# The last two blocks of a gated scan with two feed-forward layers: 480 and 480 steps in place of 512 and 448

## The chip, the cores and the metric

The kernel runs on one core of one Trainium2 chip. The metric is the device time of one execution in microseconds (us); less is better. PE is TensorE, DVE is VectorE, ACT is ScalarE, POOL is GpSimd, SP is SyncE.

## The reference, cut to what matters

Two sequences of 6080 steps with 256 channels go through a gated scan, then every step's vector goes through two feed-forward layers of width 2048.

```python
# x, f_logit: (2, 6080, 256), float32
sig = 1.0 / (1.0 + np.exp(-f_logit))
f = lower_bound + (1.0 - lower_bound) * sig
for t in range(6080):
    h = f[:, t] * h + (1.0 - f[:, t]) * x[:, t]
    y[:, t] = h
x = y.reshape(12160, 256)
h = np.maximum(x @ w_in1, 0.0)
x = h * h @ w_out1
h = x @ w_in2
g = np.where(h > 0.0, h, np.exp(np.minimum(h, 0.0)) - 1.0)
out = g @ w_out2
```

## The kernel before, in words

**Blocks.** The steps of both sequences are cut into 12 blocks, numbered 0 to 11 (`TAIL` is 11). A block holds the same stretch of steps of both sequences. Blocks 0 to 10 have 512 steps each, block 11 has the 448 that are left. Within a block the scan is done in four pieces (`pieces_of`): for each sequence the first 256 steps (`HALF`) and the rest.

**Phases.** A block goes through layer 1 in a phase `first(i)` and through layer 2 in a phase `second(i)`. The order of phases is written out by hand and is the same on every engine: `first(0), first(1), second(0), first(2), second(1), first(3), ...`, with the middle in a hardware loop, and at the end `second(8), first(10), second(9), first(11), second(10), second(11)`. The first of these phases that lie behind the loop is `second(8)`.

**Steps.** A phase has 8 steps, one for each pair of 128-wide slices of the hidden layer. In a step PE makes seven products for the current pair ("m1" to "m7", a scheme in which seven products stand for the eight of a 2x2 block product; results in four banks of PSUM, `ring`) and eight products that take the pair of two steps ago down into the sums `acc`. Each of the 15 products is a `triple` of three matmuls (line 626), because each operand is split into a high and a low part. So a step has 45 matmuls, each 128 x 128 against as many columns as the block has steps. The pieces alternate: m1, down, m2, down, and so on, with two products of `acc` side by side at the end of a step. The step of the current pair and the pair of two steps ago may belong to different phases: the first two steps of a phase take down pairs of the phase before.

**The other engines.** ACT and DVE take the seven products out of PSUM, combine and activate them and split the result (`hid_hi`, `hid_lo`); POOL helps. Phases of layer 1 also host, on DVE and ACT, the scan of the next block (`turn_f`, `turn_x`, `tanh`, `gate_x`, `scan`); `first(10)` so hosts the scan of block 11, and `first(11)` hosts none. SP loads the weights of every pair anew, the inputs, and stores the output.

**The end.** Behind `second(11)` stand the downs of the last two pairs (48 matmuls), in an order that suits what arrives last (`END_TILES`, `end_part`). Then DVE transposes `acc` into `o_sb` in five instructions (`end_turn`, line 1719) and SP and ACT store in four pieces (`end_store`, `END_PIECES`); the last of them can start only when the last transpose is done.

**Loop and block 10.** The hardware loop runs with block numbers that are not known when the program is built, and so always with 512 steps. Its last turn hosts part of the load and scan of block 10.

Of the kernel before, what the change touches and what calls it, by code (L numbers as in the profile page):

```python
# [12 lines left out]
SQ = 32  # L13
# [22 lines left out]
def gated_scan_two_ffn(nc, x, f_logit, lower_bound, w_in1, w_out1, w_in2, w_out2, out):  # L36
    B, T, D = x.shape
    F = w_in1.shape[1]
    CH = D // P
    S = BANK  # L40
    N_FULL = T // S
    TAIL = N_FULL
    S_TAIL = T - N_FULL * S
    LAST = 2 * TAIL + 1
    G = P // SQ
    ROWRUN = D // G
    assert CH == 2 and B == 2 and F == PAIRS * 2 * P
    assert HALF < S_TAIL < S and S_TAIL % SQ == 0 and N_FULL >= 4

    def known(i, block):  # L50
        return isinstance(i, int) and i == block

    def steps_of(i):
        return S_TAIL if known(i, TAIL) else S

    @dataclass
    class Phase:
# [6 lines left out]
        def n(self):  # L64
            return steps_of(self.i)
# [11 lines left out]
    def second(n):  # L77
        if known(n, TAIL):
            return Phase(2, n, LAST, PAIRS * LAST)
        return Phase(2, n, 2 * n + 2, PAIRS * 2 * n + 2 * PAIRS)  # L80
# [31 lines left out]
    def early(v):  # L112

        return isinstance(v, int) and v <= 0

    with ExitStack() as ctx:  # L116
        def sb(name, shape, dt=F32):
            return ctx.enter_context(nc.sbuf_tensor(name, shape, dt))
# [4 lines left out]
        def sem(name):  # L123
            return ctx.enter_context(nc.semaphore(name))
# [18 lines left out]
        f_raw = sb("f_raw", [P, CH * HALF])  # L143
        x_raw = sb("x_raw", [P, CH * HALF])
# [55 lines left out]
        f_loaded = sem("f_loaded")  # L200
        x_loaded = sem("x_loaded")
# [132 lines left out]
        def pieces_of(i):  # L334

            return [(b, h * HALF, min(HALF, steps_of(i) - h * HALF)) for b in range(B) for h in range(2)]
# [11 lines left out]


        END_TILES = (1, 0, 2, 3)  # L350
        MID = S_TAIL // SQ // 2
        END_PIECES = ((1, 0, MID), (1, MID, 2 * MID), (0, 0, MID), (0, MID, 2 * MID))

        END_TURNS = (1, 2, 4, 5)

# [7 lines left out]
        out_v = out.rearrange("(b t) d -> b t d", b=B)  # L363

        def end_store(eng, v, parts):

            b, k0, k1 = END_PIECES[v]
            eng.wait_ge(end_turned, END_TURNS[v])
            for a in parts:
                rows = out_v[b, TAIL * S + k0 * SQ:TAIL * S + k1 * SQ, a * ROWRUN:(a + 1) * ROWRUN]  # L370
                i = o_sb[a * SQ:(a + 1) * SQ, b, k0:k1, :, :]
                eng.dma_start(rows.rearrange("(k t) e -> t k e", t=SQ),
                              i.rearrange("t k c e -> t k (c e)")).then_inc(end_stored, DMA_INC)
# [4 lines left out]
        def _(sp):  # L378
# [11 lines left out]
            def load_rows(src, b, t0, n, dst, loaded, parts=range(G)):  # L390
                for a in parts:
                    rows = src[b, bass.ds(t0, n), a * ROWRUN:(a + 1) * ROWRUN]
                    o = dst[a * SQ:(a + 1) * SQ, 0:n * CH]
                    sp.dma_start(o.rearrange("t (k e) -> t k e", e=ROWRUN),
                                 rows.rearrange("(k t) e -> t k e", t=SQ)).then_inc(loaded, DMA_INC)

            def load_f(i, q):
                b, t0, n = pieces_of(i)[q]
                c = 4 * (i - 1) + q
                if not early(c):  # L400
                    sp.wait_ge(f_turned, c)
                load_rows(f_logit, b, i * S + t0, n, f_raw, f_loaded)

            def load_x(i, q):
                b, t0, n = pieces_of(i)[q]
                c = 4 * (i - 1) + q
                if not early(c):
                    sp.wait_ge(x_turned, c)
                load_rows(x, b, i * S + t0, n, x_raw, x_loaded)

            def raw_in_done(layer, p):

# [84 lines left out]
            def store_rows(n, b):  # L497
                S_ = steps_of(n)
                sp.wait_ge(o_n1 if b else o_n0, n + 1)
                for a in reversed(range(G)):  # L500
                    rows = out_v[b, bass.ds(n * S, S_), a * ROWRUN:(a + 1) * ROWRUN]
                    i = o_sb[a * SQ:(a + 1) * SQ, b, 0:S_ // SQ, :, :]
                    sp.dma_start(rows.rearrange("(k t) e -> t k e", t=SQ),
                                 i.rearrange("t k c e -> t k (c e)")).then_inc(out_stored[b], DMA_INC)

            def load_piece(ph, p):

                if p in (1, 4, 6) and not known(ph.i, TAIL):
                    load_f(ph.i + 1, (p + 1) // 2)
                    load_x(ph.i + 1, (p + 1) // 2)  # L510

            def phase(ph, after):
# [8 lines left out]
                for p in range(PAIRS):  # L521
                    g = ph.base + p
                    nxt = ahead(p + 2)
                    if known(ph.order, 0):
                        if p >= 1:
                            if p < PAIRS - 1:
                                load_raw_out(1, p + 1)
                            keep_q(1, p)
                            if 2 <= p < 5:
                                load_f(1, p - 1)  # L530
                                load_x(1, p - 1)
                            keep_sums(1, p - 1)
                            if p + 3 < PAIRS:
                                load_raw_in(1, p + 3)
                            elif p + 3 < PAIRS + 2:
                                load_raw_in(2, p + 3 - PAIRS)
                        if p >= PAIRS - 2:
                            load_s(nxt)
                            load_sums(nxt)
                        if p == 6:  # L540
                            load_f(2, 0)
                            load_x(2, 0)
                        continue
# [29 lines left out]
                    if before is not None and before.layer == 2:  # L573
                        if p == 2:
                            store_rows(before.i, 1)
                        if p == 3:
                            store_rows(before.i, 0)
# [36 lines left out]
            phase(second(TAIL), None)  # L614
            for v in range(len(END_PIECES)):
                end_store(sp, v, (0, 1))
            for b in range(B):
                sp.wait_ge(out_stored[b], DMA_INC * G * TAIL)
            sp.wait_ge(end_stored, DMA_INC * G * len(END_PIECES))

# [279 lines left out]
        def _(act):  # L900
# [424 lines left out]
            def end_hi_of(k):  # L1325
                act.wait_ge(end_elu, END_TILES.index(k) + 1)
                if k == 1:
                    act.wait_ge(down_n1, end.g - 1)
                if k == 2:
                    act.wait_ge(down_n0, end.g - 1)  # L1330
                nc.scalar.activation(hid_hi[:, end.par(), k, 0:end.N], end_x(end, k), ACT.Copy).then_inc(end_hi, 1)
# [8 lines left out]
            end_hi_of(3)  # L1340
            for v in range(len(END_PIECES)):
                end_store(act, v, (2, 3))

        @block.vector
        def _(dve):
# [371 lines left out]
            def end_turn(b, k0, k1, c0, c1):  # L1717

                nc.vector.transpose(o_sb[:, b, k0:k1, c0:c1, :].rearrange("p k c e -> p c k e"),  # L1719
                                    acc[:, b, c0:c1, k0 * SQ:k1 * SQ].rearrange("p c (k e) -> p c k e", e=SQ)).then_inc(  # L1720
                    end_turned, 1)

            dve.wait_ge(end_down, 1)
            dve.wait_ge(out_stored[1], DMA_INC * G * TAIL)
            end_turn(1, 0, MID, 0, CH)
            end_turn(1, MID, 2 * MID, 0, CH)
            dve.wait_ge(end_down, 2)
            dve.wait_ge(out_stored[0], DMA_INC * G * TAIL)
            end_turn(0, 0, 2 * MID, 0, 1)
            dve.wait_ge(end_down, 3)  # L1730
            end_turn(0, 0, MID, 1, CH)
            end_turn(0, MID, 2 * MID, 1, CH)

        @block.gpsimd
        def _(pool):
# [234 lines left out]
```

## Time and profile before

| | us |
|---|---|
| median of three timed runs | 1965.78 (1965.6 to 1966.9) |
| span of the profiled execution | 1963.6 |
| PE busy within the span | 1957.7 |
| DVE busy | 1604.5 |
| ACT busy | 1518.6 |
| POOL busy | 643.5 |

The span runs from the first to the last instruction of the profiled execution; the time of that execution as the timed runs count it is not listed apart. The median of the timed runs is 2.2 us more than the span, and this rest is taken as the same before and after. PE has an instruction in flight in all but 5.9 us of the span, which says that it never starves; it does not say how fast its matmuls follow one another. Matmuls overlap, so the distance between their starts is what counts, and not the duration of one.

### The profile page before, as it was taken

The numbers are of one execution on the slowest core, as the hardware profiler recorded it, in microseconds if no ns is written. First come the engines' busy times: TensorE is split into PE (matmuls) and PEld (weight loads), VectorE is DVE, ScalarE is ACT, GpSimd is POOL, SyncE is SP. The second block draws the span as 40 slices with busy tenths as digits, with TensorE's granted clock in tenths as the row PEclk, the third lists the DMA queues.
The fourth block names the chain that finished last, engine by engine and source line by source line (L and its number), as shares of the span: only waits on it lengthen the run. The fifth ranks groups of instructions, "written<-read, shape, count | busy, mean of one in ns | idle before, by whom it ended". The sixth has DMA issues, their size and how long they took to land.

```text
span 1963.6 us, 27999 instructions
## 1 busy us (share of the span) xinstructions
PE 1957.7 (100%) x8712; PEld 1632.4 (83%) x8712; DVE 1604.5 (82%) x1806; ACT 1518.6 (77%) x1848; POOL 643.5 (33%) x534
## 2 busy tenths in 40 slices
PE   9999999999999999999999999999999999999999
PEld 7888888888888888888888888888888888888888
DVE  7878887888888788888888888888888887866887
ACT  8898877877778777777777877777787777767766
POOL 4666632323223232232322323223232232332311
PEclk9999999999999999999999999999999999999999
DMA  6677453444444445344444444534434443443453
GB/s 196 204 228 227 165 150 106 148 145 127 147 135 125 130 147 146 107 148 136 126 147 142 127 124 144 147 111 150 135 119 148 145 130 113 137 136 118 140 172 112
DMA packets 228679, 281.54 MB, mean 143 GB/s; under 512 B 153857, under 2 KB 164098, under 8 KB 228610
## 3 DMA queue, kind: packets, MB, share of 16 engines
q1 hardware_dynamic: 226688, 280.23, 46.4%
q8 instruction: 35, 0.57, 0.1%
q10 hardware_dynamic: 1922, 0.46, 0.1%
q14 instruction: 34, 0.28, 0.0%
HBM read 248.25 MB, written 32.37 MB: 143 GB/s over the span
## 4 chain that ended last, share of the span: by engine, by line
PE 100%; DVE 0%; DVEq 0%; issue 0%
PE acc L626 53%; PE ring L626 46%; PE ring L663 0%; PE ring L778 0%; PE acc L785 0%; PE acc L663 0%; PE ring L785 0%; DVE o_sb L1719 0%; PE ring L823 0%; DVEq L116 0%; DVE m_sb L1632 0%
## 5 line engine op out<-in xcount | busy, mean ns | idle before, releaser
L626 PE MATMUL acc<-hid_hi,wout 128*128 128x512 f32 (+1 forms) x3072 | 1149.9, 387 | 0.0
L626 PE MATMUL ring<-t_hi,s_w 128*128 128x512 f32 (+1 forms) x2672 | 1027.3, 387 | 0.0
L626 PEld LDWEIGHTS acc<-hid_hi,wout 128*128 128x128 f32 x3072 | 576.8, 188 | 113.4 <-DMA wout<-w_kept 0.2
L626 PE MATMUL acc<-hid_lo,wout 128*128 128x512 f32 (+1 forms) x1536 | 594.7, 387 | 0.0
L626 PEld LDWEIGHTS ring<-t_hi,s_w 128*128 128x128 f32 x2672 | 501.7, 188 | 99.5 <-ACT xb L1182 0.3
L1895 POOL TENSOR_TENSOR xb<-xb,m_sb 128x512 f32<-128x512 f32 (+1 forms) x184 | 236.3, 1284 | 971.4 <-DVE hid_lo L1530 971.4
L626 PE MATMUL ring<-t_lo,s_w 128*128 128x512 f32 (+1 forms) x1336 | 517.2, 387 | 0.0
L1174 ACT ACTIVATE m_sb<-ring 128x512 f32<-128x512 f32 (+1 forms) x184 | 109.2, 593 | 354.1 <-PE ring L626 345.4
L626 PEld LDWEIGHTS acc<-hid_lo,wout 128*128 128x128 f32 x1536 | 288.4, 188 | 56.6
L626 PEld LDWEIGHTS ring<-t_lo,s_w 128*128 128x128 f32 x1336 | 250.9, 188 | 49.6
L1530 DVE TENSOR_TENSOR hid_lo<-xa,hid_hi 128x1024 fp32r<-128x1024 f32 (+1 forms) x191 | 231.3, 1211 | 61.4 <-ACT hid_hi L1153 61.2
L1530 DVE TENSOR_TENSOR hid_lo<-xb,hid_hi 128x1024 fp32r<-128x1024 f32 (+1 forms) x190 | 238.6, 1256 | 5.3 <-ACT hid_hi L1163 5.1
L1163 ACT ACTIVATE hid_hi<-xb 128x1024 fp32r<-128x1024 f32 (+1 forms) x190 | 199.0, 1047 | 38.4 <-DVE xb L1524 38.2
L1572 DVE TENSOR_TENSOR xa<-ring,u_sb 128x1024 f32<-128x1024 f32 (+1 forms) x184 | 221.7, 1205 | 0.0
L1524 DVE SCALAR_TENSOR_TENSOR xa<-ee,xa 128x1024 f32<-128x1024 f32 (+1 forms) x95 | 116.6, 1227 | 110.2 <-ACT ee L1120 110.2
L1153 ACT ACTIVATE hid_hi<-xa 128x1024 fp32r<-128x1024 f32 (+1 forms) x191 | 198.5, 1039 | 0.3
L1555 DVE TENSOR_TENSOR u_sb<-ring,m_sb 128x512 f32<-128x512 f32 (+1 forms) x184 | 123.9, 674 | 50.6 <-PE ring L626 49.4
L1561 DVE TENSOR_TENSOR u_sb<-ring,u_sb 128x512 f32<-128x512 f32 (+1 forms) x184 | 126.2, 686 | 43.9 <-PE ring L626 31.5
L1576 DVE TENSOR_TENSOR xa<-ring,xa 128x512 f32<-128x512 f32 (+1 forms) x184 | 126.3, 686 | 19.1
L1524 DVE SCALAR_TENSOR_TENSOR xb<-ee,xb 128x1024 f32<-128x1024 f32 (+1 forms) x95 | 115.4, 1214 | 23.5 <-ACT ee L1143 23.5
L1580 DVE TENSOR_TENSOR xb<-ring,u_sb 128x512 f32<-128x512 f32 (+1 forms) x184 | 123.5, 671 | 0.0
L1182 ACT ACTIVATE xb<-ring 128x512 f32<-128x512 f32 (+1 forms) x184 | 105.4, 573 | 0.0
(146 smaller groups left out, 1761.0 us busy)
## 6 DMA issues: line engine op xcount, KB each, us to landing
s_w<-s_kept SPq DMA_DIRECT2D x184, 512.0 KB, 3.8
s_w<-s_kept SPq DMA_DIRECT2D x184, 384.0 KB, 4.0
wout<-w_kept SPq DMA_DIRECT2D x88, 512.0 KB, 4.3
out_dram<-o_sb SPq DMA_DIRECT2D x88, 128.0 KB, 3.6
f_raw<-in_f_logit_dram SPq DMA_DIRECT2D x168, 64.0 KB, 3.5
x_raw<-in_x_dram SPq DMA_DIRECT2D x168, 64.0 KB, 2.7
s_kept<-ee SPq DMA_DIRECT2D x16, 512.0 KB, 4.1
s_kept<-s_w SPq DMA_DIRECT2D x8, 512.0 KB, 4.0
```

The lines of the kernel that those rows point to most:

```text
L626: mm = nc.tensor.matmul(out_ap, lhs[a], rhs[b], start=start and t == 0, stop=stop and t == 2)
L1153: nc.scalar.activation(hid_hi[:, pr.par(), 0:2, 0:N], xa[:, pr.par(), :, 0:N], ACT.Copy).then_inc(hi_n1, 1)
L1163: nc.scalar.activation(hid_hi[:, pr.par(), 2:4, 0:N], xb[:, pr.par(), :, 0:N], ACT.Copy).then_inc(hi_n0, 1)
L1174: nc.scalar.activation(m1_sb[:, 0:N], bank("m1", cur), ACT.Copy).then_inc(m1_kept, 1)
L1524: nc.vector.scalar_tensor_tensor(out=x2, in0=ee[:, v, :, 0:pr.N], scalar=1.0, in1=x2, op0=ALU.subtract, op1=ALU.max).then_inc(done, 1)
L1530: nc.vector.tensor_tensor(hid_lo[:, pr.par(), k:k + 2, 0:N], x2, hid_hi[:, pr.par(), k:k + 2, 0:N].bitcast(F32), ALU.subtract).then_inc(do ...
L1555: nc.vector.tensor_tensor(u[:, 0], bank("m6", cur), m1_sb[:, 0:N], ALU.add).then_inc(u2_done, 1)
L1561: nc.vector.tensor_tensor(u[:, 1], bank("m7", cur), u[:, 0], ALU.add).then_inc(u3_done, 1)
L1572: nc.vector.tensor_tensor(t, bank("m5", cur).unsqueeze(1).broadcast_to([P, 2, N]), u, ALU.add).then_inc(u4_done, 1)
L1576: nc.vector.tensor_tensor(t[:, 0], bank("m3", cur), t[:, 0], ALU.add).then_inc(c12_done, 1)
L1580: nc.vector.tensor_tensor(x_n0(cur)[:, 1], bank("m4", cur), u[:, 1], ALU.add).then_inc(c21_done, 1)
L1895: nc.gpsimd.tensor_tensor(t, t, m1_sb[:, 0:N], ALU.add).then_inc(c11_done, 1)
```

## The change

The numbers of steps of the last two blocks are evened out: block 10 has 480 steps instead of 512 and block 11 has 480 instead of 448. Block 11 so starts at step 5600 instead of 5632. Because 480 is 15 times 32, the four end pieces are cut as 8 and 7 groups of 32 steps instead of 7 and 7.

```diff
-    S_TAIL = T - N_FULL * S
+    S_TAIL = (T - (TAIL - 1) * S) // 2
...
     def steps_of(i):
-        return S_TAIL if known(i, TAIL) else S
+        return S_TAIL if known(i, TAIL) or known(i, TAIL - 1) else S
+
+    def start_of(i):
+        return (TAIL - 1) * S + S_TAIL if known(i, TAIL) else i * S
...
-        MID = S_TAIL // SQ // 2
-        END_PIECES = ((1, 0, MID), (1, MID, 2 * MID), (0, 0, MID), (0, MID, 2 * MID))
+        KS = S_TAIL // SQ
+        MID = (KS + 1) // 2
+        END_PIECES = ((1, 0, MID), (1, MID, KS), (0, 0, MID), (0, MID, KS))
...
-            end_turn(1, MID, 2 * MID, 0, CH)
+            end_turn(1, MID, KS, 0, CH)
...
-            end_turn(0, 0, 2 * MID, 0, 1)
+            end_turn(0, 0, KS, 0, 1)
...
-            end_turn(0, MID, 2 * MID, 1, CH)
+            end_turn(0, MID, KS, 1, CH)
```

The other edits put `start_of(i)` where `i * S` stood in the loads and stores. No instruction is added, removed or moved past another on any engine: the five instruction streams are the same before and after but for the lengths. In the phases `first(10)` and `second(10)` 512 becomes 480 (720 matmuls), in `first(11)`, `second(11)` and the end 448 becomes 480 (720 matmuls). The second scan piece of block 11 grows from 192 to 224 steps; that of block 10 is still turned and scanned with 256 steps, since this lies in the loop.

## Rows read from the trace of the kernel before

**Rows 1.** The page: span and the chain that ended last.
```profile
span 1963.6 us, 27999 instructions
PE 100%; DVE 0%; DVEq 0%; issue 0%
```

**Rows 2.** Chain of work in first(10): start, duration, what; step ends three steps apart.
```profile
1565.49 1.36 PE acc L626 x6
...
1596.09 1.36 PE acc L626 x6
```

**Rows 3.** Chain of work in second(11): step ends four steps apart.
```profile
1902.40 1.22 PE acc L626 x6
...
1938.88 1.22 PE acc L626 x6
```

**Rows 4.** Chain of work where phases meet: starts of mixed steps, and what follows.
```profile
1719.85 0.61 PE ring L626 x3
1720.46 0.69 PE acc L626 x3
...
1739.48 0.61 PE ring L626 x3
...
1794.20 0.68 PE ring L626 x3
...
1812.43 1.21 PE acc L626 x6
...
1874.87 0.61 PE ring L626 x3
...
1894.49 0.61 PE ring L626 x3
```

**Rows 5.** Timeline of PE near the start: start, time, instruction.
```profile
7.93 0.64 PE L785 MATMUL acc<-m_sb,xb 128*128 128x128 f32 x4
8.41 1.03 PE L778 MATMUL ring<-m_sb 128*128 128x512 bf16 x4
...
16.28 0.62 PE L663 MATMUL ring<-t_lo,s_w 128*128 128x512 f32 x2
...
19.50 1.07 PE L663 MATMUL acc<-t_hi,s_w 128*128 128x512 f32 x4
```

**Rows 6.** Weight loads from 1905 to 1945 us: busy us, mean ns, idle before.
```profile
L626 PEld LDWEIGHTS acc<-hid_hi,wout 128*128 128x128 f32 x70 | 13.1, 188 | 1.0
```

**Rows 7.** Busy time of each engine in three windows of first(10).
```profile
core 0: us, PE busy (x) PEld busy (x) DVE busy (x) ACT busy (x) POOL busy (x), PEclk, DMA share, GB/s
1576.60:1586.80 10.20, 10.20 (x46) 8.45 (x46) 8.18 (x10) 7.83 (x9) 4.17 (x4) 1.00 0.52 142
1586.80:1597.00 10.20, 10.20 (x46) 8.45 (x46) 10.01 (x12) 8.28 (x11) 3.99 (x4) 1.00 0.50 140
1597.00:1607.20 10.20, 10.20 (x46) 8.45 (x46) 6.53 (x9) 7.83 (x9) 3.71 (x4) 1.00 0.56 145
```

**Rows 8.** DVE in the timeline of first(10), and PE's chain after it.
```profile
1595.92 1.21 DVE L1572 TENSOR_TENSOR xa<-ring,u_sb 128x1024 f32<-128x1024 f32 x1
...
1598.81 0.68 PE ring L626 x3
```

**Rows 9.** DVE groups by form: count, busy us, mean ns, idle before.
```profile
L1572 DVE TENSOR_TENSOR xa<-ring,u_sb 128x1024 f32<-128x1024 f32 x168 | 204.4, 1217 | 0.0
L1561 DVE TENSOR_TENSOR u_sb<-ring,u_sb 128x512 f32<-128x512 f32 x168 | 116.2, 692 | 39.9 <-PE ring L626 28.3 <-issue 0.4
L1572 DVE TENSOR_TENSOR xa<-ring,u_sb 128x896 f32<-128x896 f32 x16 | 17.3, 1084 | 0.0
L1561 DVE TENSOR_TENSOR u_sb<-ring,u_sb 128x448 f32<-128x448 f32 x16 | 10.0, 622 | 4.0 <-PE ring L626 3.2
L1719 DVE STREAM_TRANSPOSE o_sb<-acc 128x448 f32<-128x448 f32 x3 | 1.8, 636 | 1.6 <-PE acc L626 1.6
L1719 DVE STREAM_TRANSPOSE o_sb<-acc 128x224 f32<-128x224 f32 x2 | 0.7, 396 | 0.0
```

**Rows 10.** The end: chain of work, then timeline.
```profile
1948.00 10.43 PE acc L626 x51
...
1951.92 0.62 DVE L1706 TENSOR_TENSOR hid_lo<-xa,hid_hi 128x448 fp32r<-128x448 f32 x1
...
1958.45 1.32 DVE L1719 STREAM_TRANSPOSE o_sb<-acc 128x448 f32<-128x448 f32 x3 [1.25 <-PE acc L626]
1958.65 0.37 PE L626 MATMUL acc<-hid_hi,wout 128*128 128x448 f32 x1
```

More of the change, by code:

```diff
@@ L48, in gated_scan_two_ffn @@
     assert HALF < S_TAIL < S and S_TAIL % SQ == 0 and N_FULL >= 4
+    assert (TAIL - 1) * S + 2 * S_TAIL == T
     def known(i, block):
@@ L369, in end_store @@
             for a in parts:
-                rows = out_v[b, TAIL * S + k0 * SQ:TAIL * S + k1 * SQ, a * ROWRUN:(a + 1) * ROWRUN]
+                rows = out_v[b, start_of(TAIL) + k0 * SQ:start_of(TAIL) + k1 * SQ, a * ROWRUN:(a + 1) * ROWRUN]
                 i = o_sb[a * SQ:(a + 1) * SQ, b, k0:k1, :, :]
@@ L401, in load_f @@
                     sp.wait_ge(f_turned, c)
-                load_rows(f_logit, b, i * S + t0, n, f_raw, f_loaded)
+                load_rows(f_logit, b, start_of(i) + t0, n, f_raw, f_loaded)
             def load_x(i, q):
@@ L408, in load_x @@
                     sp.wait_ge(x_turned, c)
-                load_rows(x, b, i * S + t0, n, x_raw, x_loaded)
+                load_rows(x, b, start_of(i) + t0, n, x_raw, x_loaded)
             def raw_in_done(layer, p):
@@ L500, in store_rows @@
                 for a in reversed(range(G)):
-                    rows = out_v[b, bass.ds(n * S, S_), a * ROWRUN:(a + 1) * ROWRUN]
+                    rows = out_v[b, bass.ds(start_of(n), S_), a * ROWRUN:(a + 1) * ROWRUN]
                     i = o_sb[a * SQ:(a + 1) * SQ, b, 0:S_ // SQ, :, :]
```

## The prediction

> **What bounds the kernel now.** I read the chain of work that ended last first. It says PE for 100% of the span [rows 1]: apart from a short start and the stores at the end, time is the sum of the distances between PE's matmuls, and every other engine waits for PE. So the question is not which engine is late, but what one matmul costs at 512, 448 and 480 columns.
>
> The chain's pieces in order of time give these distances. In the profile's rows a step ends with the only piece of six matmuls in a row, so two such pieces lie whole steps apart. In `first(10)`, with 512 columns, three steps take 1596.09 - 1565.49 = 30.60 us [rows 2], 10.20 us for 45 matmuls, 226.7 ns each. In `second(11)`, with 448 columns, four steps take 1938.88 - 1902.40 = 36.48 us [rows 3], 9.12 us for 45, or 202.7 ns each. The clock that the windows show is 1.00 [rows 7], the 2.4 GHz level; 512 columns at one per cycle would be 213.3 ns and 448 would be 186.7 ns. So a matmul carries 13.3 ns more than its columns at 512, but 16.0 ns more at 448. The overhead is not a constant, and that is what the whole sum hangs on. Were the distance a straight line in the columns, an even split would move nothing.
>
> A third reading is that of steps in which both widths alternate. The two mixed steps of `first(11)` take 1739.48 - 1719.85 = 19.63 us [rows 4]. Each has 21 matmuls of 448 and 24 of 512 columns; at the distances above that is 21 x 0.2027 + 24 x 0.2267 = 9.697 us, 19.39 for two. They are 0.24 us longer, and the rows show where: a triple of 448 takes 0.61 us as ever, one of 512 takes 0.69 instead of 0.68. The two of `second(10)` (21 of 512, 24 of 448) run from 1794.20 to 1812.43 + 1.21, 19.44 us against 19.25; those of `second(11)` from 1874.87 to 1894.49, 19.62 us against 19.39 [rows 4]. All six mixed steps together cost 0.24 + 0.19 + 0.23 = 0.66 us over the pure ones. A 512-column matmul so has a longer distance when it does not stand among its like. The same is seen near the start: 14 matmuls of 512 columns from 16.28 to 19.50 us [rows 5] take 3.22 us, 230.0 ns each, and the timeline marks no idle time ahead of these two rows. 226.7 ns is a favourable rhythm that a long run of 512s has; a run of 448s shows no equal of it.
>
> **The matmuls.** The change touches 1440 of them: 16 steps x 45 = 720 in the two phases of block 10 and as many in those of block 11. Before, they cost 720 x 0.2267 + 720 x 0.2027 = 309.1 us, plus 0.66 us in mixed steps, together 309.8 us. After, they cost 1440 x p, with p the distance at 480 columns, which no row shows. Bounds:
> - From below: 480 columns are 200.0 ns, and the least overhead seen in a long run is 13.3 ns. p = 213.3, 307.2 us. If such a rhythm also survives in the mixed steps, their 0.66 us go too: -2.6 us at most, -1.9 us if they stay.
> - From above: the price per column of the 448s, 202.7 / 448 = 0.4524 ns. p = 217.1 ns, 312.7 us, +3.5 us with the mixed steps as they are.
>
> There are six mixed steps after as before: `first(10)`, `second(9)` and `first(11)` each start with pairs of another width, while `second(10)` and `second(11)` then follow phases of their own width. So I leave the 0.66 us in. 480 lies halfway between the two widths and neither row is nearer, so I take the mean of the two prices per column, (0.4427 + 0.4524) / 2 = 0.4476 ns: p = 214.8 ns. A straight line between the two distances would give 214.7 and a change of nothing. My term is 1440 x 0.2148 = 309.3 against 309.1: **+0.2 us**.
>
> The Trainium skill ("TensorE: Matmul & The Clock Gate", section "Back-to-back issue gap") gives the distance of warm matmuls as columns over 2.4 GHz plus 2.5 ns, a straight line with a fixed overhead. By it the sum of the matmuls would not move at all, as long as the columns are the same in number. The trace does not agree with its fixed part, 13.3 and 16.0 ns here, and it is the difference of these two by which the result can move either way.
>
> **The engines beside PE.** DVE's instructions shrink in block 10 and grow in block 11, all under cover. The one tight place is the third step window of `first(10)`, where DVE hosts scan work of block 11 and is busy 10.01 us of 10.20 [rows 7]. There PE's step shrinks to 45 x 0.2148 = 9.67 us. DVE's seven pair instructions of a step shrink by half of the difference between the two forms: (1217 - 1084) / 2 = 67 ns for each of three wide ones, (692 - 622) / 2 = 35 ns for each of four narrow ones [rows 9], 0.34 us in all, while the second scan piece with 224 instead of 192 steps adds some 0.1 us. So DVE would have 9.8 us of work in a step of 9.67: late by 0.1 us. What waits for it is the next step's second product, which needs line 1572 to have read the banks: it is done at 1595.92 + 1.21 = 1597.13 and the product starts at 1598.81 [rows 8], a margin of 1.7 us. The next window has only 6.53 us of DVE work [rows 7], so the lateness is made good. Cost 0. If that cover were gone, it would be 0.1 us for each such step, at most a few tenths.
>
> In `first(11)`, `second(10)` and `second(11)` the same engines fed steps of 9.12 us without a gap; a step of 9.67 us gives them more time for their fixed costs. Cost 0.
>
> **The end.** The 54 matmuls behind the last product run without a gap (from 1948.00 [rows 10]; three records are missing). Their 24 first cover the chain of the first end tile, whose low part is ready at 1951.92 + 0.62 = 1952.54, while its matmul comes at 1948.00 + 24 x 0.2027 = 1952.86. A margin of 0.3 us. With 480 columns the 24 matmuls take 24 x 0.012 = 0.3 us more, and nine DVE and ACT instructions of that chain, at 35 to 67 ns each, 0.3 to 0.5 us more, but these start a dozen matmuls earlier, which adds another 0.15 us to PE's side. It holds, or is short by at most 0.1 us. Behind the last matmul (1958.65 + 0.37 = 1959.02) DVE is busy until 1958.45 + 1.32 = 1959.77 [rows 10]. The transposes cost (636 - 396) / 224 = 1.07 ns per column [rows 9]; 32 more columns in each of two of these three give 0.07 us. The last store has seven groups as before, the one ahead of it eight instead of seven. Together **+0.1 us**.
>
> The sum: 0.2 + 0.1 = +0.3 us on the span of 1963.6. The median of the runs shown is 1965.78, 2.2 us above the span, and I put the change on it: **1966.1 us**. A measurement of this kernel can tell about 0.2%, 3.9 us, from no change; this is far within.
>
> **The rivals.**
> - *480 finds a rhythm like that of 512* (overhead 13.3 ns). For it: 512 settles in one and stays. One mechanism that gives the same number is a floor from weight loading: each load takes 188 ns [rows 6], and 202.7 ns at 448 could be that floor and 14 ns of handing over, which 480 would clear. Against the floor: four 128-column matmuls with four weight loads take 8.41 - 7.93 = 0.48 us [rows 5], 120 ns each, so loads can come faster than every 202 ns. Sum: -1.9 to -2.6 + 0.1, **1963.3 to 1964.0 us**. Chance 0.25.
> - *480 finds none* (16 ns as for 448 up to 17.1 ns, the same price per column). For it: 448s keep that price through 16 steps, 512s out of rhythm pay nearly the same per column, 230.0 / 512 = 0.449 ns. Against: nothing but the midpoint. Sum: 1440 x (0.2160 to 0.2171) - 309.1 = +1.9 to +3.5, with the end **1967.8 to 1969.4 us**. Chance 0.3.
> - *DVE becomes the bound in `first(10)`, slower.* It decides from the point at which the lateness of 0.1 us a step adds up past the margin of 1.7 us, so if the hosted instructions grow instead of shrink with the uneven width. Eight steps in which PE then follows DVE at 10.01 instead of 9.67 us cost 2.7 us on top of any of the cases above: 1968.8 us on the middle one, over 1969.7 only on top of the dear one. Against it: the window's neighbours with 8.18 and 6.53 us. Chance 0.05.
> - *A width that is not a multiple of 64 goes like the next larger one*, 226.7 ns: 1440 x 0.012 = +17.3 us, 1983 us. No row speaks for it. Chance 0.03.
>
> **How the numbers follow.** The forecast, 1965 to 1967.5 us, has 0.34; the rivals have 0.25, 0.3, 0.05 and 0.03; 0.03 is left for a gain that I don't see. The range goes from the low end of the first rival to the high one of the second, with 0.1 us for the spread of medians on either side: 1963.2 to 1969.6 us. Faster by over 0.2% (below 1961.9) needs the unseen gain: 0.04. Slower by over 0.2% (above 1969.7) takes the last two rivals and a small part of the second: 0.11. Same: 0.85.
>
> **What the profile after would show.** Steps of 45 matmuls in `second(10)` and `second(11)` of 9.67 us if I am right, 9.60 for the first rival, 9.72 to 9.77 for the second. Mixed steps some 0.1 us over the sum of their parts. PE without idle time in `first(10)`; if there is any behind DVE, the third rival is at work. The last matmul's end to the end of the span 0.1 us longer than the 4.6 us of now. I would be wrong if the distance at 480 lay outside 213.3 to 217.1 ns.

## The result, and the profile after

The changed kernel takes 1969.31 us (median of 16 runs, 1968.73 to 1970.02) against 1965.74 us before (median of 16), 3.57 us more. One of the 16 runs before took 4027.16 us and is left out of the ratio; the median doesn't feel it. The ratio is 1.0018, with a 95% interval from 1.0011 to 1.0025. That is slower beyond its interval, but within the 0.2% that I had called "same". The range of 1963.2 to 1969.6 us holds the time. It is however not the case that I had called the likeliest, 1965 to 1967.5 us, but the second rival, no favourable rhythm at 480 columns, with 1967.8 to 1969.4 us.

The page of the profile after, with its span and PE's share, answers to [rows 1]:

```profile
span 1967.0 us, 27999 instructions
PE 1960.7 (100%) x8712; PEld 1632.5 (83%) x8712; DVE 1603.8 (82%) x1806; ACT 1518.3 (77%) x1848; POOL 642.9 (33%) x534
```

The span grew by 3.4 us, PE's busy time by 3.0. From 1500 us on the view of waits lists none for PE; DVE and ACT have as much to do as before.

The chain of work in order of time, in columns start, duration, what (line 631 is line 626 of before). A piece of six ends a step:

```profile
1555.13 1.36 PE acc L631 x6
1556.49 0.64 PE ring L631 x3
1557.14 0.70 PE acc L631 x3
1557.84 0.66 PE ring L631 x3
1558.50 0.70 PE acc L631 x3
...
1565.30 1.40 PE acc L631 x6
...
1576.87 0.65 PE ring L631 x3
...
1634.07 1.30 PE acc L631 x6
...
1654.35 1.31 PE acc L631 x6
...
1715.50 1.36 PE acc L631 x6
...
1735.84 1.40 PE acc L631 x6
...
1862.68 1.30 PE acc L631 x6
...
1940.68 1.30 PE acc L631 x6
```

From 1862.68 to 1940.68 lie eight steps of 480 columns, 78.00 us, so 9.75 us each and 216.7 ns for each of 45 matmuls. That is the number that no row of before could give. [rows 2] and [rows 3] gave 226.7 at 512 and 202.7 at 448; their middle is 214.7. 480 carries 16.7 ns on top of its 200.0, more than either neighbour.

The mixed steps became dearer too. The two of `first(10)` run from 1555.13 + 1.36 to 1576.87, 20.38 us, where 21 x 0.2167 + 24 x 0.2267 = 9.990 us twice is 19.98. Those of `second(9)`, from 1634.07 + 1.30 to 1654.35 + 1.31, take 20.29 against 19.92. Those of `first(11)`, from 1715.50 + 1.36 to 1735.84 + 1.40, take 20.38 against 19.98. Together 1.17 us over the pure ones, where [rows 4] gave 0.66. The first lines of the chain above, from 1556.49 on, show both widths at a dearer price than among their like, 0.70 us for three 512s and 0.66 for three 480s, instead of 0.68 and 0.65.

The end, from the timeline (start, time, instruction), answers to [rows 10]:

```profile
1961.52 1.40 DVE L1724 STREAM_TRANSPOSE o_sb<-acc 128x480 f32<-128x480 f32 x3 [1.35 <-PE acc L631]
...
1961.75 0.38 PE L631 MATMUL acc<-hid_hi,wout 128*128 128x480 f32 x1
```

The last matmul ends at 1962.13 and the span 4.84 us later, instead of 4.58. The three transposes take 1.40 instead of 1.32 us, but are done only 0.03 us later behind the last matmul (0.78 instead of 0.75). The other 0.23 us lie behind them, in the stores.

The account: 1440 x (216.67 - 214.67) ns = 2.88 us for the distances, 0.51 us for the mixed steps, 0.3 us for the end, 3.7 us. The spans differ by 3.4: this execution was already 0.16 us ahead at 1534 us, before the first changed matmul, and 0.1 us is left as rounding.

And the tight place that [rows 7] showed, in windows of the changed kernel cut at its steps (busy us and count by engine):

```profile
core 0: us, PE busy (x) PEld busy (x) DVE busy (x) ACT busy (x) POOL busy (x), PEclk, DMA share, GB/s
1576.87:1586.61 9.74, 9.74 (x46) 8.45 (x46) 7.70 (x10) 7.45 (x9) 3.93 (x5) 1.00 0.53 150
1586.61:1596.37 9.76, 9.76 (x47) 8.46 (x46) 9.58 (x11) 8.01 (x11) 3.65 (x4) 1.00 0.53 144
1596.37:1606.11 9.74, 9.74 (x46) 8.44 (x46) 6.58 (x9) 7.45 (x9) 3.89 (x5) 1.00 0.61 150
```

DVE is busy 9.58 of 9.76 us in the second of them, and PE doesn't wait.

### The profile page after: what moved, and what is told of

It is laid out like the page before. It is cut to its first block, busy times and chain, and to the rows that moved or that the text cites. A ratio compares the mean times of both kernels' runs of the same rounds, so it can differ in the third digit from the quotient of the medians.

```text
span 1967.0 us, 27999 instructions
## 1 busy us (share of the span) xinstructions
PE 1960.7 (100%) x8712; PEld 1632.5 (83%) x8712; DVE 1603.8 (82%) x1806; ACT 1518.3 (77%) x1848; POOL 642.9 (33%) x534
## 4 chain that ended last, share of the span: by engine, by line
PE 99%; DMA 0%; DVE 0%; SPq 0%; ACT 0%; DVEq 0%; issue 0%
PE acc L631 53%; PE ring L631 46%; PE ring L668 0%; PE acc L790 0%; DMA xa<-in_f_logit_dram 0%; PE acc L668 0%; DVE o_sb L1724 0%; PE ring L783 0%; SPq L393 0%; ACT xa L1217 0%; DVEq L120 0%
```

## The experiments

The theory after the result: the loss lies in TensorE alone, as the price that a matmul of fp32r data has at each width when it follows others of its kind (Theory A); fp32r is the 4-byte type in which the kernels hand TensorE its operands. The rivals: the engines around it, the transfers, or a floor set by the weight loads.

**Widths alone.** A kernel with nothing but matmuls on PE, each with its own weight load, into eight banks of PSUM that no engine reads: 60 of bf16, then 90 of each width in fp32r (120 of 512), then bf16 again at three widths. An entry of `STAGES` such as `("f", (480,), 90)` is 90 fp32r matmuls of 480 columns.

```python
for kind, ns, count in STAGES:
    for q in range(count):
        n = ns[q % len(ns)]
        o = ring[:, v % 8, 0:n]
        if kind == "f":
            mm = nc.tensor.matmul(o, wts[:, v % 4, :], mov[:, v % 2, 0:n], start=True, stop=True)
        ...
        v += 1
```

> TensorE alone: runs of 90 matmuls of one width each, every one with its own weight load, nothing reading PSUM, no other engine. It computes nothing of the reference. Theory A (the distance is a property of the width itself, of fp32r streaming): 512 columns settle at 226.7 ns, 480 at 216.7, 448 at 202.7, as in the kernel, and bf16 lies near the columns over 2.4 GHz, some 13 ns lower. Theory B (the distance comes from the surroundings: engines reading PSUM and SBUF, waits on semaphores): all widths lie on one straight line here, 480 halfway between 448 and 512. Theory C (weight loading is a floor near 200 ns): 416, 384 and 320 columns stay at about 200 ns.

Five of the groups of PE by form (count, busy us, mean ns of one):

```profile
L80 PE MATMUL ring<-mov,wts 128*128 128x504 f32 x90 | 20.6, 388 | 0.0
L80 PE MATMUL ring<-mov,wts 128*128 128x496 f32 x90 | 20.3, 385 | 0.0
L80 PE MATMUL ring<-mov,wts 128*128 128x480 f32 x90 | 19.7, 378 | 0.0
L80 PE MATMUL ring<-mov,wts 128*128 128x448 f32 x90 | 18.4, 365 | 0.0
L80 PE MATMUL ring<-mov,wts 128*128 128x256 f32 x90 | 11.0, 283 | 0.0
```

Busy time is 90 distances and one overhang of about 0.16 us. Taken from the starts of successive matmuls in the trace, over the second half of each run:

| columns | 512 | 504 | 496 | 488 | 480 | 472 | 464 | 456 |
|---|---|---|---|---|---|---|---|---|
| distance, ns | 226.7 | 226.7 | 223.3 | 220.0 | 216.7 | 213.3 | 208.9 | 208.9 |
| over columns / 2.4 GHz | 13.3 | 16.7 | 16.7 | 16.7 | 16.7 | 16.7 | 15.6 | 18.9 |

| columns | 448 | 440 | 432 | 416 | 384 | 320 | 256 |
|---|---|---|---|---|---|---|---|
| distance, ns | 202.7 | 200.0 | 196.1 | 188.4 | 173.3 | 146.7 | 120.0 |
| over columns / 2.4 GHz | 16.0 | 16.7 | 16.1 | 15.1 | 13.3 | 13.3 | 13.3 |

The three distances of the kernels come out to a tenth of a nanosecond with no other engine at work, which refutes Theory B. Theory C falls as well: 256 columns take 120.0 ns, so there is no floor near 200 from the weights. The 128-column matmuls of [rows 5], each with its weight load, stand at 120 ns too; if the loads set a floor, it lies no higher than that.

480 is not the odd one out. From 504 down to 472 the overhead is 16.7 ns throughout. 512 is cheaper than its neighbours, its last 8 columns cost nothing. But it is not alone with its 13.3 ns: 384, 320 and 256 columns have them too. Of the multiples of 64 that were measured only 448, the other width of the kernel before, stands higher, at 16.0, and the scan of places further down finds 448 with 13.3 ns as well, from another start.

The bf16 matmuls took 215 to 217 ns at 512, 202.5 at 480 and 189.2 at 448 columns. This is what the Trainium skill ("TensorE: Matmul & The Clock Gate", section "Back-to-back issue gap") states for the isolated gap of warm matmuls, columns over 2.4 GHz plus 2.5 ns; the trace agrees for bf16 and does not for fp32r.

**Widths in turn.** The same kernel with alternating widths, for instance `("f", (480,)*3 + (512,)*3, 120)`.

> TensorE alone: runs in which widths alternate, three and three as in the mixed steps, singly, and one odd matmul in sixteen. It computes nothing of the reference. Theory A (512 has a favourable rhythm that another width breaks, 480 has a lesser one): three 480s and three 512s cost 5 ns or more over the mean of the pure distances, 221.7 ns, per matmul; one 480 in sixteen makes its fifteen 512s cost 230 ns for some matmuls each time; 448 with 512 costs about 2.5 ns over the mean of 214.7. Theory B (surroundings): every mix costs the mean of its parts.

Measured, as the mean distance over the 120 or 160 matmuls of a sequence, beside the mean of the pure distances:

| sequence | measured | mean of pure |
|---|---|---|
| three 480, three 512 | 226.5 | 221.7 |
| three 448, three 512 | 217.1 | 214.7 |
| three 480, three 448 | 210.1 | 209.7 |
| 480, 512 singly | 223.5 | 221.7 |
| 448, 512 singly | 218.7 | 214.7 |
| fifteen 512, one 480 | 228.7 | 226.0 |
| fifteen 480, one 512 | 217.8 | 217.3 |

Theory A holds, though 4.8 ns came where 5 or more were expected. 45 x 4.8 ns = 0.22 us is what a mixed step of 480 and 512 should cost more, and the changed kernel shows 0.19 to 0.20; for 448 and 512 it is 45 x 2.4 = 0.11, and [rows 4] give 0.10 to 0.12. After a lone 480 nine matmuls of 512 took 224 to 236 ns each before they stood at 226.7 again. 480 among 448s costs next to nothing: most of the loss is that of 512's rhythm.

**The other order.** Block 10 with 448 steps, block 11 with 512, all work done.

```diff
-    S_TAIL = (T - (TAIL - 1) * S) // 2
+    S_TAIL = S
+    S_NEXT = T - (TAIL - 1) * S - S_TAIL
...
-        return S_TAIL if known(i, TAIL) or known(i, TAIL - 1) else S
+        return S_NEXT if known(i, TAIL - 1) else S
...
-        return (TAIL - 1) * S + S_TAIL if known(i, TAIL) else i * S
+        return (TAIL - 1) * S + S_NEXT if known(i, TAIL) else i * S
```

> Block 10 has 448 steps and block 11 has 512: the widths of before in the other order, all work done. Theory A (the price is that of each width): 720 matmuls at 226.7 and 720 at 202.7 ns as before, eight mixed steps instead of six (+0.2 us), and an end with 512 columns, twice the 0.3 us that the end of the changed kernel gained: 1966.3 to 1966.8 us, clearly under the 1969.3 of two times 480. Rival D (first(10) with narrower steps lets DVE, busy 10.01 of 10.20 us there, become the bound; with 480 too): TensorE shows idle time in first(10), whose steps of 9.12 us leave DVE 0.9 us short, and the time is 1968 us or more. Rival E (what the last block's phases and the end cost grows with its width, not the width's own price): well over 1969.3 us.

1966.32 us (11 runs, 1965.97 to 1966.66) against 1965.61 for the kernel before: Theory A. The same 960 steps cost 0.7 us more than before when cut as 448 and 512, and 3.6 us more when cut as 480 and 480. Rivals D and E are gone with it. `first(10)` here has steps of 9.12 us, and a window cut at the tight one shows DVE busy for 9.01 of them, with PE still at work without a gap:

```profile
1585.58:1594.70 9.12, 9.12 (x47) 8.47 (x46) 9.01 (x11) 7.86 (x11) 3.35 (x4) 1.00 0.56 157
```

**PE's widths of before in the changed kernel.** Only TensorE's columns are put back: block 10 gets 32 stale ones more, and the last 32 steps of block 11 are left out of both layers.

```diff
+            def cols(pr):
+                for i, n in ((TAIL - 1, 512), (TAIL, 448)):
+                    if known(pr.phase.i, i):
+                        return n
+                return pr.N
...
-                mm = triple(acc[:, n, c, 0:pr.N], [w[:, h, c * P:(c + 1) * P] for h in range(2)],
-                            [t[:, pr.par(), k, 0:pr.N] for t in (hid_hi, hid_lo)],
+                mm = triple(acc[:, n, c, 0:cols(pr)], [w[:, h, c * P:(c + 1) * P] for h in range(2)],
+                            [t[:, pr.par(), k, 0:cols(pr)] for t in (hid_hi, hid_lo)],
...
```

The seven products into `ring` and the matmuls of the end take `cols` in the same way.

> The changed kernel (480 and 480 steps on ACT, DVE, POOL and in all transfers), but TensorE's matmuls have the widths of before: 512 columns for block 10 (32 stale ones more), 448 for block 11 (the last 32 steps of it are left out of both layers). Theory A (the whole loss lies in TensorE's distances at 480 columns and in its mixed steps): steps of 10.20 and 9.12 us again, the time falls from 1969.3 back to 1965.6 to 1966.2 us, of which up to 0.3 us are the longer transposes and stores. Rival B (the other engines' 480-step work or its transfers slow TensorE down): it stays at 1968 us or more.

1966.50 us (11 runs, 1966.09 to 1967.10) against 1965.65. 2.8 of the 3.6 us are back, but it misses my bracket by 0.3 us. The trace says why. From the 2000th matmul to the 8670th PE runs like the kernel before, at a constant 0.09 us ahead of it. Then, in the end, a gap opens (timeline of PE):

```profile
1952.43 0.36 PE L631 MATMUL acc<-hid_hi,wout 128*128 128x448 f32 x1
1953.30 0.44 PE L631 MATMUL acc<-hid_hi,wout 128*128 128x448 f32 x1 [0.51 <-DVE hid_lo L1718]
```

The starts are 0.87 us apart instead of 0.20. The other engines' chain for the first end tile is that of 480 steps, PE's 24 matmuls of cover are those of 448, and the margin of 0.3 us that I had read from [rows 10] is overdrawn. At the last matmul PE is 0.71 us behind the kernel before, and the transposes and stores of 480 columns add the 0.3 us that they cost the changed kernel too. The gap is an effect of this experiment alone: the changed kernel covers the chain with 480 columns and shows no such gap.

**472 columns in the changed kernel.** The same edit with 472 for both blocks; the last 8 steps of each are left out.

> The changed kernel with TensorE at 472 instead of 480 columns for both blocks (the last 8 steps of each are left out of both layers); the other engines as in the changed kernel. Theory A: 1440 matmuls fall from 216.67 to 213.33 ns as in the lone scan, steps from 9.75 to 9.60 us, 4.8 us in all: 1964.5 us. Rival B (DVE or another engine holds the pace at 9.75 us a step): under 2 us faster, with idle time on TensorE.

1963.81 us (11 runs, 1963.34 to 1965.05), 5.5 us under the changed kernel where 4.8 were expected. The chain of work in `second(10)` and `second(11)`:

```profile
1859.40 1.28 PE acc L631 x6
...
1936.20 1.28 PE acc L631 x6
```

76.80 us for eight pure steps, 9.60 each, 213.3 ns a matmul as in the lone scan, PE without idle time. The 0.7 us beyond are the mixed steps: those of `first(10)` take 9.98 us each where the pure distances give 9.92, so all six cost about 0.3 us over the pure ones and not 1.17. The time follows PE's distance.

**504 columns in the kernel before.** TensorE takes 504 of block 10's 512 columns, by the same `cols`.

> The kernel before, but TensorE takes only 504 of 512 columns in its matmuls for block 10 (the last 8 steps of that block are left out of both layers). Theory A (504 costs what 512 costs, as in the lone scan of widths, 226.7 ns both): the same 1965.6 us within 0.5. Rival L (in the kernel time goes with the columns): 720 matmuls times 8 columns at 0.375 to 0.417 ns make it 2.2 to 2.4 us faster, 1963.3 us.

1965.87 us (11 runs, 1965.58 to 1967.57) against 1965.65: the same. 720 matmuls with 8 columns fewer gave nothing; the pure steps of `first(10)` stay at 10.20 us:

```profile
1598.36 1.36 PE acc L626 x6
...
1608.56 1.36 PE acc L626 x6
```

What moved are mixed steps: those of 504 with 512 take 10.33 us each instead of 10.20, and those of 504 with 448 are cheaper by 0.06 to 0.08 us each than those of 512 with 448.

**The end pieces.** 7 and 8 groups instead of 8 and 7, in the changed kernel: `MID = KS // 2` instead of `(KS + 1) // 2`.

> The changed kernel with the four end pieces cut as 7 and 8 groups instead of 8 and 7; all work done. Theory A (the end's growth by 0.3 us over before comes from its sizes as a whole): the last transpose grows by 32 columns (0.03 us) and the last store by an eighth, the one before shrinks: within 0.2 us of 1969.3. Rival (the third store's size delays the last one): 0.2 to 0.4 us faster.

1969.09 us (11 runs, 1968.67 to 1970.50): 0.2 us less than the median of the changed kernel, within the spread of either. It doesn't tell the two apart.

**What the overhead hangs on.** Matmuls alone again, with weights of 128, 64 and 32 columns and with a shifted start of the moving operand.

> TensorE alone, runs of 90 matmuls; it computes nothing of the reference. Weight loads are narrowed from 128 to 64 and 32 columns, the moving operand keeps its 512, 480 or 448 columns, and for 480 it also begins 8, 16 and 32 columns further on. Theory A1 (what comes on top of the columns, 13.3, 16.7 and 16.0 ns, belongs to the weight load that runs beside the matmul): it shrinks with narrower weights, towards 215.8, 202.5 and 189.2 ns, the bf16 distances. Theory A2 (it belongs to streaming 4-byte columns): 226.7, 216.7 and 202.7 stay at every width of the weights. Theory A3 (alignment of the stretch read): 480 columns change with the offset.

The mean distances in ns, over the second half of each run:

| weights | 512 | 480 | 448 |
|---|---|---|---|
| 128 columns | 226.7 | 216.7 | 202.7 |
| 64 columns | 230.0 | 216.7 | 202.2 |
| 32 columns | 231.7 | 220.0 | 202.2 |

The records of a weight load shrink from 188 ns to 134 and 108, and no distance falls by more than 0.5 ns, where Theory A1 wanted 11 to 14 ns less. So A1 falls, and what is left is the streaming of 4-byte columns, which no run takes apart further. But with narrower weights 512 loses its rhythm. And the start counts: 480 columns from 8, 16 and 32 on took 220.0, 218.3 and 220.0 ns, so A3 is right as well, and A2, by which the distances stay at every width of the weights, is not the whole of it.

**Places.** A scan of starts and spacings of the moving operand.

> TensorE alone, runs of 60 matmuls; it computes nothing of the reference. The moving operand's 448 or 480 columns begin 0 to 64 columns further on in two buffers 512 columns apart, or the buffers lie 448, 480, 544 or 960 columns apart, or there is only one. Theory S (each matmul streams at a price that only its number of columns sets, and the start shifts the phase): 448 gives 202 to 204 ns and 480 gives 216 to 220 ns at every place. Rival P (the place of the operand relative to a boundary in SBUF decides): some place gives 448 columns in 200.0 ns or 480 in 213.3, which would be worth 1.9 us in the kernel before or 4.8 us in the changed one, and the kernel could be laid out so.

Mean distances again over the second half of each run, in ns, of 448 columns by the start:

| start | 0 | 8 | 16 | 24 | 32 | 40 | 48 | 56 | 64 |
|---|---|---|---|---|---|---|---|---|---|
| distance, ns | 202.7 | 206.7 | 200.0 | 205.3 | 204.0 | 206.7 | 202.2 | 204.4 | 206.7 |

480 columns took 216.7 ns from 0 and 220.0 from 24. With buffers at 32 and 544 they took 213.3 ns, where the kernel above had 220.0 for the same two starts; there the buffers lie elsewhere in SBUF and another run stands ahead, and no run tells which of the two makes the difference. Buffers 448, 480 or 960 columns apart, or a single one, changed nothing (202.7 and 216.7 ns); with 544 between them 512 columns took 230.0 ns, 480 took 215.1 and 448 took 203.3. The windows over the runs of 60 at starts 0 and 16 (after the length: busy us and count of PE, PE's weight loads, ACT and POOL, then clock and DMA):

```profile
39.28:51.45 12.17, 12.17 (x61) 11.27 (x60) 0.00 (x0) 0.00 (x0) 1.00 0.19 64
63.84:75.85 12.00, 12.00 (x61) 11.25 (x60) 0.00 (x0) 0.00 (x0) 1.00 0.00 0
```

The rival P is right: 448 columns from 0 took 202.7 ns in all three runs of this kernel that begin there, whatever stood ahead of them, and the other starts move the distance by up to 7 ns. From 16 the 448 carry 13.3 ns over their columns, from 8, 40 and 64 they carry 20.0.

**The two places tried in the kernels.** All of the work is done; only the columns in which ACT, DVE and POOL put TensorE's moving operands change, in `t_hi`, `t_lo`, `hid_hi` and `hid_lo`.

```diff
+    def at_of(i):
+        return 16 if known(i, TAIL) else 0
...
-                nc.scalar.activation(t_hi[v][:, 1:3, 0:N], raw_of(ph)[:, 1, :, 0:N], ACT.Copy).then_inc(t_hbb, 1)
+                nc.scalar.activation(t_hi[v][:, 1:3, at_of(ph.i):at_of(ph.i) + N], raw_of(ph)[:, 1, :, 0:N], ACT.Copy).then_inc(t_hbb, 1)
```

> The kernel before (512 and 448), all work done, with the moving operands of block 11 (t_hi, t_lo, hid_hi, hid_lo) begun at column 16 of their 512-column slots instead of column 0. Theory P (what the lone runs showed holds here: 448 columns from 16 on take 200.0 ns instead of 202.7): steps of 9.00 instead of 9.12 us in block 11's pure steps, 720 x 2.67 ns = 1.9 us less, 1963.7 us. Rival (with other weights, destinations and neighbours 448 settles in another rhythm): 202 to 204 ns, within 1 us of 1965.6.

1964.39 us (11 runs, 1963.95 to 1964.77) against 1965.69 (21 runs, 1965.29 to 1967.12). The ratio is 0.9992, its interval from 0.9983 to 1.0001; it just reaches 1, so by the ratio alone the two can't be told apart, while every run lies under every run of the kernel before and the trace shows where the time went. The chain of work in `second(11)`:

```profile
1901.64 1.20 PE acc L629 x6
...
1937.64 1.20 PE acc L629 x6
```

36.00 us for four steps, 9.00 each, 200.0 ns a matmul where [rows 3] have 202.7. So this place carries over from the lone run. 1.9 us were expected and 1.3 came, because the mixed steps with 512 cost 1.1 us instead of 0.66.

> The changed kernel (480 and 480), all work done, with the moving operands of both blocks begun at column 32. The lone runs gave two answers for this place, 219.9 and 213.4 ns. Theory P with the lower one: 1440 x 3.3 ns = 4.8 us less, 1964.5 us. With the higher one: 1440 x 3.2 ns = 4.6 us more, 1973.9 us. Rival (the place has no part in it): 1969.3 us.

1969.61 us (11 runs, 1969.13 to 1970.98): neither time of Theory P. By the time alone the rival, that the place has no part in it, would hold, since the changed kernel takes 1969.31. The trace refutes it:

```profile
1864.40 1.31 PE acc L634 x6
...
1942.80 1.31 PE acc L634 x6
```

PE's pure steps are 9.80 us, 217.8 ns a matmul instead of 216.7, while its mixed steps cost nothing extra (20.03 us for two of `first(10)`, and 20.03 by the pure distances). 0.05 us more in each of 32 steps and 1.2 us less in mixed ones nearly cancel. What a place gives can't be carried over blindly.

## Why the prediction came out as it did

- **What bounds the kernel**: right. PE paces every step, and its distances at 480 columns, with their surroundings in mixed steps, make up 3.4 of the 3.7 us of the account. Putting PE's widths back alone brought 2.8 of 3.6 us back, and 472 columns gave 5.5.
- **The price at 480 columns**: the term that was mis-sized. I took the mean of the two prices per column, 214.8 ns, between 213.3 and 217.1. It is 216.7, so +2.9 us instead of +0.2. That is 2.7 of the 3.2 us by which the forecast of 1966.1 missed. The bounds on the distance held and gave the range its upper end, 1969.4 for a measured 1969.31. That the sum held as well is in part luck: the mixed steps and the end came out 0.7 us dearer than it has them, and the distance lay 0.5 ns under its bound, worth 0.7 us, so that two misses cancelled. The step that failed is "480 lies halfway and neither row is nearer": I treated the 13.3 ns of 512 and the 16.0 ns of 448 as two samples of one slowly changing thing, and the scan shows that it doesn't change slowly: 13.3, 16.7, 15.6, 18.9 and 16.0 ns between 512 and 448. The rows already said that 512's can't be counted on, since [rows 4] and [rows 5] showed it lost among other widths, and 512 columns out of rhythm at 230.0 ns [rows 5] carry 230.0 - 213.3 = 16.7 ns, to the tenth what 480 then measured. To take the overhead of a matmul without the rhythm, which is the second rival, would have made 1968 to 1969 the likeliest case. Nothing in the rows proved that 480 would have it.
- **The mixed steps**: six as counted, but I left their 0.66 us as they were without a reason; they cost 1.17. The lone runs give 4.8 ns a matmul for 480 with 512 against 2.4 for 448 with 512.
- **DVE in the tight step** (the fourth step of `first(10)`, not the third as I called it): the cost of nothing is right, the lateness is not. Computed were 9.8 us of work in a step of 9.67, measured 9.58 in 9.76, so DVE isn't late; with steps of 9.12 us there was no wait on PE either.
- **The end**: +0.1 us was said, +0.3 measured. The transposes grew by 0.08 us where 0.07 were worked out, but only 0.03 of it shows behind the last matmul; the time behind the transposes, which I had left as it was, gave 0.23. That the first end tile's chain is covered was right, and the experiment with PE's old widths shows the point from which it doesn't.
- **The rivals**: 480 with the 13.3 ns of 512 didn't come by itself; one lone run has it, at another place in SBUF, and the kernel with its operands from column 32 doesn't. The floor from weight loading is refuted by 120.0 ns at 256 columns and by the narrow weights. The width that counts as the next larger one doesn't exist at 480, but does between 504 and 512.
- **The chances**: "same" by 0.2% is where the measured 0.18% falls, close to its edge. The case that came had 0.3, the forecast 0.34.

The price at each width is measured, in the kernels and alone. Its cause stays open: what it is in the streaming of fp32r columns that makes 13.3 ns at one place and width and 16.7 or 20 at another. Width, start in SBUF, weights' width and the matmuls before all have a part; no run isolates a boundary or a period.

## What to carry to other kernels

When one engine paces a kernel at a hundred per cent and a change leaves the total of its work alone, the price of one instruction at the new size is the whole question, and it is cheap to measure by itself: a run of 90 matmuls gave the number to a tenth of a nanosecond. Don't interpolate between two sizes unless a third shows that the price runs smoothly between them; if a size loses its price among neighbours, expect a new size to have the price without it. Even shares are not better in themselves: here 512 and 448, in either order, beat 480 and 480, and mixing widths step by step has a price of its own.

## What the runs showed of the hardware that was not expected

- fp32r matmuls at a granted clock of 1.00 stand at 226.7 ns for 504 columns as for 512, and at 208.9 for 456 as for 464; from 504 down to 472 it is 3.3 ns for every 8 columns. Over their columns 512, 384, 320 and 256 carry 13.3 ns, 504 to 472 carry 16.7, 448 carries 16.0 from column 0.
- The distance depends on where the moving operand starts: 448 columns from column 16 of a slot take 200.0 ns instead of 202.7, in a lone run and in the kernel, where all the work is done in 1964.39 us, 1.3 us under the kernel before (interval of the ratio 0.9983 to 1.0001).
- Fifteen 512s with a 480 between them average 228.7 ns where their parts average 226.0; widths 512 and 448 in turn cost 218.7 instead of 214.7.
- Narrower weights (64 or 32 columns) make fp32r matmuls of 512 columns slower, 230.0 and 231.7 ns instead of 226.7, while the weight loads' own records get shorter, 134 and 108 ns instead of 188.
